# Attention, experts and a dense layer on one core: routing batch by batch, sorted rows into the dense stage, transposed scores, a state read over the whole array

## The reference

```python
# x: 8 batches x 8 heads x 512 rows x 64; state: 8 x 8 x 32 x 64 (all float32)
scores = scale * x @ state.T;  a  = exp(scores - max);  a  /= a.sum(-1) + 1e-9;   xread = a @ state
scores2 = scale * state @ x.T; a2 = exp(scores2 - max); a2 /= a2.sum(-1) + 1e-9;  sread = a2 @ x
x = concat([xread, sread], axis=2).transpose(0, 2, 1, 3).reshape(8 * 544, 512)
# experts: one of 8 for each row, w1[e] is 512 x 1024, w2[e] is 1024 x 512
xn = x / (norm(x) + 1e-6); en = emb / (norm(emb) + 1e-6); logits = xn @ en.T / tau
expert = argmax(logits); gate = softmax(logits)[expert]
x = gate * (relu(x @ w1[expert]) @ w2[expert])
# dense: w_in is 512 x 2048, w_out is 2048 x 512
out = (s * relu(x @ w_in) ** 2 + b) @ w_out
```

## Time and profile before

| | us |
|---|---|
| median of 3 runs (lowest to highest) | 1500.07 (1498.54 to 1501.28) |
| span of the profiled execution | 1499.6 |
| PE: a matmul in flight | 1396.4 |
| PEld: a weight load in flight | 1160.5 |
| DVE busy | 534.1 |
| ACT busy | 509.6 |
| POOL busy | 193.3 |

### The profile page before, as it was taken

How to read it: one execution, slowest core, us unless ns; L and a number is a source line. 1 busy time by engine, 2 the same in 40 slices (tenths; PEclk the granted TensorE clock), 3 DMA queues, 4 the chain that set the end, 5 groups by cost and what they waited for, 6 DMA issues and landing times.

```text
span 1499.6 us, 20856 instructions
## 1 busy us (share of the span) xinstructions
PE 1396.4 (93%) x6774; PEld 1160.5 (77%) x6775; DVE 534.1 (36%) x801; ACT 509.6 (34%) x882; POOL 193.3 (13%) x251
## 2 busy tenths in 40 slices
PE   6999518999999999999499999999999999999998
PEld 5888406888888888887488888888888888888886
DVE  3566681144422144131632232323323232232322
ACT  4677502244433244243232222222222222222221
POOL 1111331222222222221600000000000000000000
PEclk7999758999999999999699999999999999999999
DMA  8677313124432124213101010100101010010000
GB/s 208 177 199 224 103 15 141 42 100 152 148 142 104 42 93 150 98 36 147 47 1 42 1 56 0 56 0 0 56 0 56 0 47 9 0 56 0 29 1 28
DMA packets 88456, 105.22 MB, mean 70 GB/s; under 512 B 44262, under 2 KB 59622, under 8 KB 87921
## 3 DMA queue, kind: packets, MB, share of 16 engines
q1 hardware_dynamic: 82160, 85.52, 18.3%
q0 software_dynamic: 6272, 19.41, 3.8%
HBM read 78.15 MB, written 27.80 MB: 71 GB/s over the span
## 4 chain that ended last, share of the span: by engine, by line
PE 51%; DVE 1%; DVEq 0%; issue 0%; ACT 0%
PE ps_g L1404 25%; PE ps_o L1422 25%; PE ps_yt L1392 1%; DVE w_out_lo L1367 1%; DVE w_raw L1360 0%; DVE g_lo L1350 0%; DVE y_lo L1339 0%; PE ps_o L1440 0%; DVE sq L1347 0%; DVEq L1449 0%; ACT rel L1311 0%; DVEq L1363 0%
## 5 line engine op out<-in xcount | busy, mean ns | idle before, releaser
L1347 DVE TENSOR_TENSOR sq<-rel 128x512 f32<-128x512 f32 (+1 forms) x144 | 97.3, 676 | 492.7 <-ACT rel L1311 492.6
L1311 ACT ACTIVATE rel<-ps_g 128x512 f32<-128x512 f32 (+1 forms) x144 | 82.8, 575 | 534.4 <-PE ps_g L1404 534.4
L1404 PE MATMUL ps_g<-y_hi,w_in_hi 128*128 128x512 f32 (+1 forms) x576 | 218.8, 380 | 3.7 <-DVE y_lo L1339 3.6
L1404 PE MATMUL ps_g<-y_lo,w_in_hi 128*128 128x512 f32 (+1 forms) x576 | 218.2, 379 | 0.0
L1404 PE MATMUL ps_g<-y_hi,w_in_lo 128*128 128x512 f32 (+1 forms) x576 | 218.1, 379 | 0.0
L1422 PE MATMUL ps_o<-w_out_hi,g_hi 128*128 128x512 f32 x544 | 213.4, 392 | 0.6 <-DVE g_lo L1350 0.6
L1422 PE MATMUL ps_o<-w_out_lo,g_hi 128*128 128x512 f32 x544 | 211.9, 389 | 0.0
L1422 PE MATMUL ps_o<-w_out_hi,g_lo 128*128 128x512 f32 x544 | 211.7, 389 | 0.0
L1404 PEld LDWEIGHTS ps_g<-y_hi,w_in_hi 128*128 128x128 f32 x576 | 109.3, 190 | 25.3 <-DVE y_lo L1339 4.0
L1404 PEld LDWEIGHTS ps_g<-y_lo,w_in_hi 128*128 128x128 f32 x576 | 109.3, 190 | 20.6 <-issue 0.2
L1404 PEld LDWEIGHTS ps_g<-y_hi,w_in_lo 128*128 128x128 f32 x576 | 109.3, 190 | 20.0
(11 more groups left out here) (215 smaller groups left out, 1737.7 us busy)
## 6 DMA issues: line engine op xcount, KB each, us to landing
w_raw<-in_moe_w SPq DMA_DIRECT2D x16, 2048.0 KB, 9.7
out_rows<-w_raw SPq DMA_DIRECT2D x34, 256.0 KB, 2.1
x_a<-in_x SPq DMA_DIRECT2D x8, 1024.0 KB, 7.4
x_tok<-x_rows SPq DMA_DIRECT2D x8, 1024.0 KB, 5.5
y_rows<-moe_tok SPq DMA_DIRECT2D x8, 1024.0 KB, 5.6
x_m<-in_x SPq DMA_DIRECT2D x7, 1024.0 KB, 9.5
w_raw<-in_moe_w_out SPq DMA_DIRECT2D x1, 4096.0 KB, 14.9
w_raw<-in_moe_w_in SPq DMA_DIRECT2D x1, 3072.0 KB, 14.3
```

What stands on the lines that cost most here:

```text
L1311: nc.scalar.activation(rel[:, k, 0:cols], ps_g[k][:, 0:cols], ACT.Relu).then_inc(rel_ready, 1)
L1347: nc.vector.tensor_tensor(sq[:, 0:cols], rel[:, k, 0:cols], rel[:, k, 0:cols], ALU.mult).then_inc(sq_ready, 1)
L1404: last = nc.tensor.matmul(ps_g[n % 2][:, 0:cols], w[:, wc], a[:, c, 0:cols], start=(c == 0 and w is w_in_hi and a is y_hi), stop=(c == DC ...
```

## The change

Attention: scores are computed transposed at once (state stationary, 64 columns in one half of the array; x_t streamed, 512 columns), and turned back for the token direction. The embeddings are folded in for each pair of heads in turn: `x_rows` and `st_rows` are 544 columns wide (4 pairs of 128 and 8 logits each), and go to `x_tok` with their logits. The state read takes `a2_n`, 128 stationary columns of which each 32 are one head, and 256 columns of x. The token read uses 64 rows of the array for each pass (`read_bank[..][par]`). The loop is unrolled, and a batch's second half runs behind the next batch's scores. Each batch is routed at once: VectorE chooses (`choose`), TensorE ranks rows within experts (`ranks`), VectorE adds the expert's base, a fixed region of the table per expert (`place`), and GpSimd scatters the row numbers into `slot_tab` in DRAM, five scatters a batch.

Experts: each tile's indices are loaded from `slot_tab`, the row numbers kept in sorted order in `moe_id`, and the gate is computed per tile from the gathered logits (`gate_scale`, `gate_soft`, `gate_square`, with a reciprocal root in small VectorE steps) and applied to the output. `yg` is stored in sorted order. w_in's split moves to the changes of expert; w1[0] and w2[0] are split in attention. The last tile's `down` runs after the dense rows' first transposes.

Dense: rows come sorted and gated; w_out is split block by block, four blocks ahead (AHEAD), within the first group; results are scattered to `out` by row number on GpSimd. `line_pad` fills the tiles of the whole program up to a multiple of 128 bytes of a partition, and the expert block's index tiles stand behind the large ones.

The core of the diff (`@@` names the engine; `RW` is 544, `HP` 64, `CAP` the slots of an expert's region):

```diff
+x_tok = nc.dram_tensor("x_tok", [NTOK, RW], f32, kind="Internal").ap()
+slot_tab = nc.dram_tensor("slot_tab", [ZCOLS * P, 1], i32, kind="Internal").ap()
+moe_tok = nc.dram_tensor("moe_tok", [NTOK + 4 * P, D], f32, kind="Internal").ap()
+moe_id = nc.dram_tensor("moe_id", [NTOK + 4 * P, 1], i32, kind="Internal").ap()
-x_tok = nc.dram_tensor("x_tok", [NTOK, D], f32, kind="Internal").ap()
-gate_tok = nc.dram_tensor("gate_tok", [NTOK, 1], f32, kind="Internal").ap()
-moe_tok = nc.dram_tensor("moe_tok", [NTOK, D], f32, kind="Internal").ap()
...
+    sb(top, "line_pad", [P, (-(-used // 128) * 128 - used) // 4], f32)
...
-    xg = sb(mo, "xg", [P, D], f32)
-    xg_in = sb(mo, "xg_in", [P, D], f32)
-    g_idx0 = sb(mo, "g_idx0", [P, 1], i32)
-    g_idx = sb(mo, "g_idx", [P, 1], i32)
-    s_idx = sb(mo, "s_idx", [P, 1], i32)
-    xg_hi = sb(mo, "xg_hi", [P, D], f32r)
+    xg_hi = sb(mo, "xg_hi", [P, D], f32r)
...
@@ SP @@
+for bb in range(B):
+    if bb + 3 < B:
+        load_x(bb + 3)
+    sp.wait_ge(rows_ready, 2 * TPB * (bb + 1))
+    sp.dma_start(x_dst(bb), x_rows[:]).then_inc(rows_stored, 16)
+    sp.wait_ge(log_ready, bb + 1)
+    sp.dma_start(x_tok[bb * ROWS + S:bb * ROWS + ROWS, :], st_rows[:]).then_inc(st_stored, 16)
+for e in range(1, E):
+    sp.wait_ge(w1_ready, WS * e)
+    sp.dma_start(w_raw[:, 0:WCOLS], w1[e].rearrange("(c p) n -> p c n", p=P)).then_inc(w1_loaded, 16)
+    sp.wait_ge(win_ready, e)
+    load_win(e)
+    sp.wait_ge(w2_ready, WS * e)
+    sp.dma_start(w_raw[:, WCOLS:2 * WCOLS], w2[e].rearrange("(c p) n -> p c n", p=P)).then_inc(w2_loaded, 16)
...
@@ GpSimd: slots, experts, out @@
+pool.wait_ge(tab_zero, 4)
+pool.wait_ge(tab_cleared, 16)
+for bb in range(B):
+    pool.wait_ge(pos_ready, bb + 1)
+    for t in range(TPB + 1):
+        n = P if t < TPB else NS
+        nc.gpsimd.indirect_dma_start(out=slot_tab[:, :],
+                                     out_offset=bass.IndirectOffsetOnAxis(ap=pos5[0:n, t:t + 1], axis=0),
+                                     in_=ids[0:n, bb, t:t + 1], in_offset=None).then_inc(slots_written, 16)
...
+def tile_ids(g, first):
+    if not first:
+        pool.wait_ge(gathered, 16 * g)
+        pool.wait_ge(id_stored, 16 * g)
+    pool.dma_start(g_idx[:], slot_tab[0:P, :] if first else slot_tab[ds(slots_of(pool, g), P), :])\
+        .then_inc(idx_loaded, 16)
+    pool.wait_ge(idx_loaded, 16 * g + 16)
+
+def gather(g):
+    nc.gpsimd.indirect_dma_start(out=xg[:], out_offset=None, in_=x_tok[:, :],
+                                 in_offset=bass.IndirectOffsetOnAxis(ap=g_idx[:], axis=0)).then_inc(gathered, 16)
+
+def keep_ids(g):
+    pool.dma_start(moe_id[ds(rows_of(pool, g), P), :], g_idx[:]).then_inc(id_stored, 16)
+
+def next_tile(g):
+    tile_ids(g, False)
+    keep_ids(g)
+    pool.wait_ge(tab_ready, 1)
+    pool.wait_ge(xg_tr, g)
+    pool.wait_ge(gate_sq, g)
+    pool.wait_ge(gate_lg, g)
+    gather(g)
+
+def store(g):
+    pool.wait_ge(yg_ready, g + 1)
+    if not starts(g):
+        pool.wait_ge(moe_stored, 16 * g)
+    pool.dma_start(moe_tok[ds(rows_of(pool, g), P), :], yg[:]).then_inc(moe_stored, 16)
...
+with pool.Fori(1, last) as g:
+    next_tile(g + 3)
+    store(g)
...
+        nc.gpsimd.indirect_dma_start(out=out[:, :],
+                                     out_offset=bass.IndirectOffsetOnAxis(ap=out_id[:, r:r + 1], axis=0),
+                                     in_=o_sb[:, k, :], in_offset=None).then_inc(o_stored, 16)
...
@@ ScalarE: order in a batch, order in a tile @@
+for i in range(B):
+    for jj in range(2):
+        act.wait_ge(scT_done, 2 * i + jj + 1)
+        if i >= 1:
+            act.wait_ge(scN_done, i)
+        nc.scalar.activation(s_t[:, jj, :], bank_t[jj][:], ACT.Copy).then_inc(sT_ready, 1)
+    for jj in range(2):
+        act.wait_ge(nb_done, 2 * i + jj + 1)
+        if i >= 1:
+            act.wait_ge(e2_tr, 2 * i)
+            act.wait_ge(sum2_steps, 2 * i)
+        nc.scalar.activation(e2[:, jj, :], s_t[:, jj, :], ACT.Exp, bias=nb2[:, jj:jj + 1], scale=-1.0,
+                             accum_out=s2[:, jj:jj + 1]).then_inc(e2_done, 1)
+    if i + 1 < B:
+        for j in range(PAIRS):
+            x_evac(i + 1, j)
+    act.wait_ge(sh_done, i + 1)
+    nc.scalar.activation(e1[:], e1[:], ACT.Exp, scale=-1.0).then_inc(e1_done, 1)
+    split_hi(i)
+    if i >= 1:
+        row_t_evac(i - 1)
+    for jj in range(2):
+        act.wait_ge(e2_tr, 2 * i + jj + 1)
+        if i >= 1:
+            act.wait_ge(sread_done, i)
+        nc.scalar.activation(a2_n[:, :, jj * P:(jj + 1) * P], bank_t[jj][:].rearrange("p (t w) -> p t w", w=P),
+                             ACT.Copy).then_inc(a2_ready, 1)
+    if i >= 1:
+        rows_evac(i - 1)
+row_t_evac(B - 1)
+rows_evac(B - 1)
...
+def tile(g):
+    hidden(g + 1)
+    x_hi(g + 2)
+    next_w1(g + 1)
+    result(g)
+    gate_soft(g + 2)
+    act.wait_ge(gate_ready, g + 3)
+    gate_square(g + 3)
+    hidden_hi(g + 1)
+    next_w2(g)
...
@@ VectorE @@
+def token_rows(bb):
+    dve.wait_ge(sread_done, bb + 1)
+    dve.wait_ge(sum2_steps, 2 * bb + 2)
+    if bb >= 1:
+        dve.wait_ge(st_stored, 16 * bb)
+        dve.wait_ge(row_tr, bb)
+    for q in range(P // NS):
+        par, hh = q // 2, q % 2
+        p = slice(NS * q, NS * q + NS)
+        nc.vector.tensor_tensor(
+            st_rows[:, par * 2 * GW:(par + 1) * 2 * GW].rearrange("n (j w) -> n j w", j=2)[:, :, hh * DH:hh * DH + DH],
+            bank_r[p].rearrange("p (j w) -> p j w", j=2)[:, :, q * DH:q * DH + DH],
+            r2[p, :].unsqueeze(2).to_broadcast([NS, 2, DH]), ALU.mult).then_inc(st_rows_ready, 1)
...
+def place(bb):
+    dve.wait_ge(rank_mm, bb + 1)
+    route_step(nc.vector.tensor_tensor(rk5[:], bank_l[:, L_RANK:L_RANK + (TPB + 1) * E]
+                                       .rearrange("p (t e) -> p t e", e=E), hot5[:], ALU.mult))
+    route_step(nc.vector.tensor_reduce(rank5[:], rk5[:], X_AXIS, ALU.add))
+    route_step(nc.vector.scalar_tensor_tensor(rank5[:], pick5[:], -float(CAP), rank5[:], ALU.mult, ALU.add))
+    if bb >= 1:
+        dve.wait_ge(slots_written, 16 * (TPB + 1) * bb)
+    nc.vector.tensor_scalar(pos5[:], rank5[:], float(E * CAP), None, ALU.add).then_inc(pos_ready, 1)
...
+def choose(bb):
+    tail = [P, TPB + 1, E]
+    dve.wait_ge(rows_ready, 2 * TPB * (bb + 1))
+    route_step(nc.vector.tensor_reduce(lg5[:, 0:TPB, :],
+                                       x_rows[:].rearrange("p t (q w) -> p t w q", q=PAIRS)[:, :, P:P + E, :],
+                                       X_AXIS, ALU.add))
+    route_step(nc.vector.tensor_reduce(top5[:], lg5[:], X_AXIS, ALU.max))
+    route_step(nc.vector.tensor_tensor(hit5[:], lg5[:], top5[:].unsqueeze(2).to_broadcast(tail), ALU.is_ge))
+    route_step(nc.vector.tensor_tensor(hit5[:], hit5[:], order[:], ALU.mult))
+    route_step(nc.vector.tensor_reduce(pick5[:], hit5[:], X_AXIS, ALU.max))
+    route_step(nc.vector.tensor_tensor(hot5[:], order_m[:], pick5[:].unsqueeze(2).to_broadcast(tail), ALU.is_equal))
+    if bb >= 1:
+        route_step(nc.vector.tensor_copy(pre5[:, 0, :], pre5[:, TPB + 1, :]))
+    for t in range(TPB + 1):
+        ins = nc.vector.tensor_tensor(pre5[:, t + 1, :], pre5[:, t, :], hot5[:, t, :], ALU.add)
+        if t < TPB:
+            route_step(ins)
+        else:
+            ins.then_inc(hot_ready, 1)
...
+def gate_scale(g):
+    n_gate = [0]
+
+    def gate_link(ins):
+        n_gate[0] += 1
+        ins.then_inc(gate_step, 1)
+        dve.wait_ge(gate_step, GATE_STEPS * g + n_gate[0])
+
+    dve.wait_ge(gathered, 16 * g + 16)
+    nc.vector.tensor_reduce(lg[:], xg[:].rearrange("p (q w) -> p w q", q=PAIRS)[:, P:P + E, :], X_AXIS, ALU.add)\
+        .then_inc(gate_lg, 1)
+    dve.wait_ge(gate_lg, g + 1)
+    gate_link(nc.vector.tensor_reduce(gc[:, 3:4], lg[:], X_AXIS, ALU.max))
+    gate_link(nc.vector.tensor_scalar(sh[:], lg[:], gc[:, 3:4], None, ALU.subtract))
+    dve.wait_ge(gate_sq, g + 1)
+    rsqrt_steps(gate_link, gc[:, 4:5], gc[:, 5:6], gc[:, 0:1], gc[:, 4:5].bitcast(i32), gi[:, 0:1])
+    gate_link(nc.vector.tensor_tensor(gc[:, 6:7], gc[:, 0:1], gc[:, 4:5], ALU.mult))
+    gate_link(nc.vector.tensor_scalar(gc[:, 6:7], gc[:, 6:7], NORM_EPS, None, ALU.add))
...
+def tile(g):
+    x_lo(g + 2)
+    next_w1(g + 1)
+    gate_final(g + 2)
+    hidden_lo(g + 1)
+    next_w2(g)
+    gate_scale(g + 3)
...
@@ TensorE @@
+def scores(i):
+    pe.wait_ge(xt_ready, PAIRS * (i + 1))
+    pe.wait_ge(st_ready, B // 2 if i else 2)
+    if i >= 1:
+        pe.wait_ge(a2_ready, 2 * i)
+    for jj in range(2):
+        for par in range(2):
+            p = slice(HP * par, HP * par + HP)
+            last = nc.tensor.matmul(bank_t[jj][p, :], st_t[:, i, jj, p], x_t[:, 2 * jj + par, :], start=True, stop=True)
+        last.then_inc(scT_done, 1)
...
+def state_read(bb):
+    pe.wait_ge(a2_ready, 2 * bb + 2)
+    if bb >= 1:
+        pe.wait_ge(st_rows_ready, (P // NS) * bb)
+    for jj in range(2):
+        for t in range(TPB):
```

(76 more changed lines are left out.)

1688 lines of the change are left out of this document (720 added, 968 removed).

## The result

The changed kernel takes 1686.88 us (1684.35 to 1688.66, 4 runs) against 1499.3 for the kernel before (4 runs): a ratio of 1.124 (95% interval 1.123 to 1.126). The forecast was 1442, the range 1380 to 1474. The profiled execution's span is 1682.9 us.

What follows compares the result with a forecast made beforehand. TensorE bounds the kernel except where it lacks work, mainly routing, which VectorE bounds. Terms -36.7 + 5 + 3 - 13.5 - 18.6 + 2.5 = -58.3 on 1499.6 give 1441.3, forecast as 1442 us; range 1380 to 1474.

Steps and rivals of the forecast that it cites:

- the chain of the feed: Experts: yg, store, index load, keep_ids and gather take 10.2 us from a tile's end, needed at 13.5: 3.3 us cover.
- feed late: Rival, experts: index load and gather each land in 6.8 us, chain 2.9 late 37 times: +107, 1549 us; chance 0.05.
- Who interferes with whom: Skill rule: VectorE's two-port mode shuts GpSimd out, so gate steps would lengthen the feed's chain; no own size or chance.
- Changes of expert: At seven changes, gate steps behind VectorE's weight splits hold the next gather about 0.4 us: +3.
- its product is wanted 7.2 after, behind up: nothing: Experts: ScalarE's wait for gate_ready holds hidden_hi until 2.5 us after the tile's end, at no cost.
- The start: Start of the experts: three feed chains follow each other, turn_x(2) waits 3.6 us and the clock may fall: +5.
- To the first expert matmul: Attention and routing: last e1 transposes end at 159.4, then 33.2 us, so experts start at 192.6: -36.7.
- Halves of the array: Attention: score and token_read passes in different array halves run in pairs at once, scores 1.7 us instead of 3.4.
- Rate of the experts: Expert matmuls go from 0.234 to 0.227 us apart because big tiles stand on multiples of 128 bytes: -13.5.
- The full rate of 0.215: Rival: experts and dense stage both at 0.215 us a matmul, 1382 us; chance 0.14.
- Into the dense stage: From last hidden transposes to first full dense group: 62.8 us instead of 81.4, -18.6.
- Tail: End of the kernel: GpSimd scatters in place of SP's stores take 7.9 us for 5.4, +2.5.

Runs made afterwards that it cites:

- e1: Changed kernel with the write of row numbers (keep_ids) issued behind the gather, not ahead of it: 1596.44 us, ratio 1.065.
- e2: Changed kernel with the row-number write still ahead of the gather, but as one contiguous 512-byte piece from slot_tab in DRAM: 1553.39 us, ratio 1.035.
- e4: Kernel before, with a write of the tile's 128 indices, 4 bytes per partition, added ahead of every gather: 1494.17 us (one run).
- e16: e15 with row numbers again written as 128 pieces of 4 bytes from the index tile ahead of each gather: 1664.04 us, ratio 1.109.
- e15: e13 with VectorE's gate steps cut in two, only the first ahead of w2's split, the other 14 behind: 1487.84 us, ratio 0.991.
- e13: e2 plus indices a turn earlier, gate steps before w2's split, attention's splits at batch end, new order around expert changes: 1505.81 us, ratio 1.004.
- e14: e13 with 12 unused float32 matmuls a batch added on TensorE in attention: 1505.58 us.
- (6): Placement runs: kernel before with tiles padded, 1498.38 and 1496.57 us; e2 with early indices and gate steps first, tiles moved off 128-byte multiples, 1560.77 us.

## Why the prediction was wrong, point by point

**The failed step** is the chain of the feed: "From a tile's end: yg 0.8, store issue 1.0, index load 3.7, keep_ids issue 1.0, gather 3.7: 10.2, ... 3.3 us of cover." keep_ids was priced by its issue on GpSimd alone. What it does on the way to memory, 128 pieces of 4 bytes ahead of the gather, was priced at nothing, and the gather behind it at the median of gathers that had nothing of the kind in front. Runs e1, e2, e4 and e16 show it from four sides: 9.6 to 10.2 us with the write ahead, 3.5 to 3.6 without. Writing the row another way gives back 125 us of the experts (e2), and the old write costs 176 (e16). With 9.8 for 3.7 the chain is 16.3 and 2.8 us late a tile, 37 times: +104. Two more of its terms were off, and in part cancel: the index load lands in 2.3 us (median), not 3.7, but the steps between the DMAs take more than was priced. In the turn shown above the tile ends at 309.8 and the gather starts at 318.1: 8.3 us, where the chain has 6.5.

The rival "feed late" (0.05) had this place and nearly this lateness, by another way (both landings at 6.8, the longest gather; the gather's median is now above it, the index load far below). Its chance was the mistake, and its 1549 is still 138 us short. The trace of before had a hint in the earlier trace rows: the load of gate_rows, one word per row, takes 5.3 us. It was used for the index load and not for the write.

The Trainium skill, "DMA: Bandwidth & Descriptors", Specifications, says that below 512 bytes the DMA engines read, modify and write. The runs don't show this to be the cause: in the packet records the write is 16 packets of 32 bytes in the changed kernel and in e2 alike, and the index loads, of such packets too, land in 2.3 us. What in the write holds up the gather, the number of its pieces or the index tile as its source, stays open. The rule of "SBUF — State Buffer", Who interferes with whom, in the Trainium skill, weighed as a rival, isn't borne out: the issue stayed at 1007 ns, and the landing came back with the gate's steps in place.

**The rest of the +205** was in three further terms. Changes of expert were put at +3; in e2, with a fast gather, each of the seven still costs 9 us in its first two tiles and some 1.5 in a third, in e15 about 3. That "its product is wanted 7.2 after, behind up: nothing" held within a tile, but not where 4.9 us of splits stand ahead of gate and hidden_hi on ScalarE and 5.8 on VectorE: e13 and e15 took most of the cost away by order alone. The start was put at +5: the first two distances between tiles are 53.3 us in the changed kernel and 35.5 in e2, for 23.2 before. And as TensorE waits, its clock falls: 0.89 in 500:600, for 1.00 in the earlier trace rows, so that `up` behind a late gather takes 6.55 to 7.7 us for 5.7.

**To the first expert matmul**: -18.2 for -36.7. The last transposes of the tile e1 end at 170.4, not 159.4. A batch took 19.7 us, not 18.0, at a clock of 0.87. The term that the runs point to is the clock, taken as 1.00: e14 at 1.00 takes 18.5, with 2.6 us of added matmuls, and e15 and e16, with the splits at a batch's end, 16.7 and 17.5 near it. From there the way to the first matmul was 40.7 us for 33.2; the last of the slots' scatters alone is 7.4 us from its issue to the index load.

**Halves of the array**: right. The score passes start in pairs 7 ns apart, eight of them in 1.9 us at full clock in e15; those of the token read, in row halves, do so too, 0.116 us a pair (the changed kernel):

```profile
81.97 0.62 PE L1164 MATMUL bank_a<-st_pair,a_t 64*128 64x136 f32 x6
```

**Rate of the experts**: 0.227 was right, and its reason half right (6); 38 x 48 x 0.0075 is 13.7, not 13.5. The full rate of 0.215 didn't come; the fp32r matmuls reach it in no run here.

**Into the dense stage**: -12.0 for -18.6, the mechanism right and three sizes too small. The last `down` starts 4.6 us after the hidden transposes (4.0), and takes 7.0 with its first matmuls 0.43 us apart (5.6). In the first group VectorE, with w_out's split in between, takes 4.5 us a step (squares at 908.5, 913.0, 917.5) where 3.2 were taken, so that from there to the full group it is 57.8 us for 53.2.

**Tail**: +8.0 for +2.5. The last scatter is issued 5.4 us after the last matmul, 1.3 after the one before it, where 4.2 were worked out; it lands after 2.7 where 3.7 were taken, at 1677.6. What ends last is something that the sum doesn't have, GpSimd's closing DRAIN, 5.0 us behind that landing:

```profile
L1369 POOLq DRAIN  x1: 9782/9782/9782, 1672.8 to 1672.8; - x1
```

In the kernel before GpSimd had long drained (746.2, 1.5 us).

**State read**: no gain, as forecast (16 passes, 3.7 us, for 3.62 before).
